# Token numbers from the chip, another order on SP's queue, fewer count reads, and one group's sums on VectorE, in a fused attention, expert and FFN kernel

## The reference

```python
def phi(x):                                  # x: batch 4, heads 8, seq 576, dim 64
    proj = einsum('bhsd,df->bhsf', x, w_phi)             # 128 features
    proj = proj - max(abs(proj), -1)
    return concatenate([exp(proj), exp(-proj)], -1)
kv = einsum('bhsf,bhsd->bhfd', phi(k), v); z = sum(phi(k), 2)
attn = phi(q) @ kv / (phi(q) . z + 1e-6)                 # -> x (2304, 512)

e_idx = argmax(x @ w_gate, 1)                            # one of 8 experts per token
out[e_idx == e] = softmax prob * sigmoid(x @ w_output_gate)[e] * (relu(x @ w1[e]) @ w2[e])   # 1024 wide

xn = x / sqrt(mean(x*x) + 1e-6) * rms_g                  # FFN, 1536 wide
y = (silu(xn @ w_gate) * (xn @ w_val)) @ w_out
```

## Time and profile before

| | |
|---|---|
| median of 3 runs | 870.38 us (868.96 to 873.25) |
| the profiled execution | 873.63 us, span of the trace 871.9 us |
| busy, share of the span | PE 96%, PEld 87%, DVE 62%, ACT 40%, POOL 19% |
| granted TensorE clock, mean | 0.998 |
| moved by DMA | 122.41 MB, 140 GB/s |

### The profile page before, as it was taken

The page is one execution under the profiler, slowest core; times in us unless marked ns, Lnnn a source line. Parts: engine busy times, 40 slices in busy tenths (PEclk is TensorE's granted clock), DMA queues, the critical chain, the costliest instruction groups (busy, mean ns, idle before and its releaser), DMA issues.

```text
span 871.9 us, 16594 instructions
## 1 busy us (share of the span) xinstructions
PE 840.2 (96%) x6216; PEld 757.3 (87%) x6217; DVE 538.9 (62%) x934; ACT 347.3 (40%) x547; POOL 161.4 (19%) x169
## 2 busy tenths in 40 slices
PE   8999999998988999999989999999999999999997
PEld 6685867767988999999989999999999998888885
DVE  5688786989766954445569777666765774212210
ACT  4544454573155533322354443333433443212211
POOL 1010302112350433203421031111110000101101
PEclk9999999999999999999999999999999999999999
DMA  8613713112349544554662852232421945343320
GB/s 285 209 57 138 275 54 108 55 38 75 127 175 267 227 114 97 141 148 150 184 230 77 280 180 79 79 80 79 142 71 54 357 150 184 123 139 125 125 101 36
DMA packets 65226, 122.41 MB, mean 140 GB/s; under 512 B 9200, under 2 KB 43120, under 8 KB 62480
## 3 DMA queue, kind: packets, MB, share of 16 engines
q1 hardware_dynamic: 57600, 91.98, 34.3%
q0 software_dynamic: 3488, 17.85, 5.3%
q10 hardware_dynamic: 4080, 11.80, 3.9%
HBM read 77.54 MB, written 44.09 MB: 139 GB/s over the span
## 4 chain that ended last, share of the span: by engine, by line
PE 78%; DVE 11%; issue 6%; DMA 2%; ACT 1%; DVEq 1%; SPq 0%; another core or an unknown queue 0%; POOLq 0%; POOL 0%; ACTq 0%
PE ps L1207 9%; PE ps L1209 9%; PE ps L1208 9%; PE ps L1259 5%; PE ps L1258 5%; PE ps L1260 5%; PE ps L956 3%; PE ps L1115 3%; PE ps L1116 3%; PE ps L1117 3%; PE ps L1128 3%; PE ps L1130 3%; PE ps L1129 3%; PE ps L1011 3%; PE ps L916 2%
## 5 line engine op out<-in xcount | busy, mean ns | idle before, releaser
L1207 PE MATMUL ps<-sH,tb 128*128 128x384 f32 x504 | 171.0, 339 | 5.9 <-DVE val L2018 2.9
L1208 PE MATMUL ps<-sL,tb 128*128 128x384 f32 x504 | 170.0, 337 | 0.0
L1209 PE MATMUL ps<-sH,tb 128*128 128x384 f32 x504 | 169.9, 337 | 0.0
L1207 PEld LDWEIGHTS ps<-sH,tb 128*128 128x128 f32 x504 | 95.0, 189 | 8.5 <-DVE val L2018 4.9
L1208 PEld LDWEIGHTS ps<-sL,tb 128*128 128x128 f32 x504 | 95.1, 189 | 0.1
L1209 PEld LDWEIGHTS ps<-sH,tb 128*128 128x128 f32 x504 | 95.2, 189 | 0.0
L2036 DVE TENSOR_TENSOR hTL<-h_st,hTH 128x768 fp32r<-128x768 f32 x36 | 33.0, 954 | 97.4 <-ACT hTH L1516 97.4
L1260 PE MATMUL ps<-woH,hTL 128*128 128x512 f32 x216 | 84.1, 389 | 0.0
L1259 PE MATMUL ps<-woL,hTH 128*128 128x512 f32 x216 | 84.1, 389 | 0.0
L1258 PE MATMUL ps<-woH,hTH 128*128 128x512 f32 x216 | 84.0, 389 | 0.0
L1115 PE MATMUL ps<-xmH,w1H 128*128 128x288 f32 x256 | 76.8, 300 | 5.9 <-issue 2.8
(11 more groups left out here) (246 smaller groups left out, 1784.8 us busy)
## 6 DMA issues: line engine op xcount, KB each, us to landing
h_dram<-hid SPq DMA_DIRECT2D x36, 384.0 KB, 2.8
h_st<-h_dram SPq DMA_DIRECT2D x18, 768.0 KB, 4.1
t_dram<-tb SPq DMA_DIRECT2D x6, 1792.0 KB, 5.7
t_raw<-in_ffn_up SPq DMA_DIRECT2D x13, 512.0 KB, 3.2
tb<-t_dram ACTq DMA_DIRECT2D x6, 1024.0 KB, 6.7
xin<-xs_dram SPq DMA_DIRECT2D x9, 578.2 KB, 9.3
xs_dram<-zrow SPq DMA_DIRECT2D x8, 578.2 KB, 7.9
qT<-in_q SPq DMA_DIRECT2D x4, 1152.0 KB, 5.8
```

What stands on the lines that cost most here:

```text
L1207: e.matmul(to, wh, xh, start=(fresh and c == 0), stop=False, skip_group_check=True)
L1208: e.matmul(to, wh, xl, start=False, stop=False, skip_group_check=True)
L1209: done = e.matmul(to, wl, xh, start=False, stop=(c == 1), skip_group_check=True)
```

## The change

1. Token numbers: `numbers_out` now takes the step's numbers from `xin` on the chip (96 partitions x 3 values of 4 bytes) instead of from `xs_dram`, as soon as the step's rows have been loaded. `rows_next` waits until the last numbers have been stored, since it overwrites `xin`. The two number transfers in the FFN's units 8 and 10 go.
2. SP's order in a step: rows in, FFN weights out, numbers out, normalised rows out, next FFN weights in.
3. Hand-over: group 0's rows are loaded ahead of the operands of visit 0; those of visit 1 wait for VectorE's first operand `s_hi0`. In unit 4 the last rows' store and group 2's load go ahead of the store of the unit's hidden rows.
4. Loop ends: counts of both turns are read at the head of a pair, and the first step (on VectorE also the next count) only inside a turn that has steps.
5. GpSimd loads the next raw `w1` ahead of `gate_rows`. Group 2's sums are VectorE's, in units 7 and 8.

```diff
+SUM_AT = {(1, "A"): ((1, 0), (1, 1)), (1, "B"): ((1, 2), (1, 3)), (7, "B"): ((2, 0), (2, 1)), (8, "A"): ((2, 2),),
+          (8, "B"): ((2, 3),)}
...
-        def turn_of(e, x):
-            tiles = e.value_load(tab[0:1, bass.ds(x + TILES, 1)], min_val=0, max_val=NTOK // G)
-            first = e.value_load(tab[0:1, bass.ds(x + FIRST, 1)], min_val=0, max_val=NTOK // G + E)
-            return tiles, first
+        def turns_of(e, pair):
+            return [e.value_load(tab[0:1, bass.ds(pair * 2 + (par + TILES), 1)], min_val=0, max_val=NTOK // G)
+                    for par in range(2)]
+        def first_of(e, x):
+            return e.value_load(tab[0:1, bass.ds(x + FIRST, 1)], min_val=0, max_val=NTOK // G + E)
...
             with e.Fori(0, pairs) as pair:
-                for par in range(2):
-                    tiles, first = turn_of(e, pair * 2 + par)
+                counts = turns_of(e, pair)
+                for par, tiles in enumerate(counts):
                     with e.If(tiles > 0):
+                        first = first_of(e, pair * 2 + par)
                         if once is not None:
                             once(pair, par)
...
+            def numbers_out(n, col):
+                e.wait_ge(s["ld"], n * 16 + 16)
+                settle(e, "carry_sp")
+                e.wait_ge(s["idst"], n * 16 + 16)
+                settle(e, "carry_sp")
+                with nc.allow_non_contiguous_dma(reason="token numbers"):
+                    e.dma_start(ids_dram[bass.ds(col, G), :].rearrange("(t p) a -> p t a", p=GR), xin[:, :, DM:DM + 1])\
+                        .then_inc(s["idst"], 16)
...
                 rows_in(x0 * REGION)
+                numbers_out(0, 0)
                 e.wait_ge(s["pe_XT"], KC)
+                e.wait_ge(s["idst"], 32)
                 rows_in(x0 * REGION + G)
...
                 row = row_of(n)
                 e.wait_ge(s["pe_XT"], n * KC)
                 settle(e, "carry_sp")
-                rows_in(row)
-            def numbers_out(n, col, row):
                 e.wait_ge(s["idst"], n * 16 + 16)
                 settle(e, "carry_sp")
-                with nc.allow_non_contiguous_dma(reason="token numbers"):
-                    e.dma_start(ids_dram[bass.ds(col, G), :], xs_dram[bass.ds(row, G), DM:DM + 1])\
-                        .then_inc(s["idst"], 16)
+                rows_in(row)
             def rows_out(n, col):
...
             with e.If(early < 1):
                 e.sem_inc(s["e_st"], 16)
                 rows_in(row_of(0))
+                numbers_out(0, column_of(0))
                 step_weights_in(0)
                 rows_next(1)
                 weights_out(0)
                 step_weights_in(1)
+            numbers_out(1, column_of(1))
             with e.Fori(0, total - 2) as n:
                 rows_next(n + 2)
                 weights_out(n + 1)
+                numbers_out(n + 2, column_of(n + 2))
+                rows_out(n, column_of(n))
                 step_weights_in(n + 2)
-                col, row = column_of(n), row_of(n)
-                rows_out(n, col)
-                numbers_out(n, col, row)
             rows_next(total)
...
             settle(e, "carry_sp")
-            e.wait_ge(s["e_st"], 16 * 8)
-            operands_in(0)
             e.wait_ge(s["xst"], total * 16)
             settle(e, "carry_sp")
             group_in(0)
-            prior_col, prior_row = column_of(prior), row_of(prior)
-            rows_out(prior, prior_col)
-            e.wait_ge(s["pe_s1"], total * FC)
-            settle(e, "carry_sp")
+            e.wait_ge(s["e_st"], 16 * 8)
+            operands_in(0)
+            rows_out(prior, column_of(prior))
+            e.wait_ge(s["s_hi0"], 1)
             operands_in(1)
             e.wait_ge(s["pe_s2"], total * FC + 2)
             settle(e, "carry_sp")
             group_in(1)
             e.wait_ge(s["s_lo"], 5)
             operands_in(2)
-            last_col, last_row = column_of(last), row_of(last)
+            last_col = column_of(last)
             for u in range(NU):
-                hidden_out(u)
                 if u == ROOT_AT + 1:
                     rows_out(last, last_col)
                     e.wait_ge(s["s_lo"], 7)
                     e.wait_ge(s["xst"], total * 16 + 32)
                     settle(e, "carry_sp")
                     group_in(2)
+                hidden_out(u)
                 for vis in MADE:
                     if last_of_visit(vis - 3) == u + 1:
                         weights_in(vis)
-                if u == 8:
-                    numbers_out(prior, prior_col, prior_row)
-                if u == 10:
-                    numbers_out(last, last_col, last_row)
                 if u == 15:
                     e.wait_ge(s["idst"], total * 16 + 16)
                     settle(e, "carry_sp")
...
             def split_step(pair, par, g):
                 add_squares(g - 1)
+                with e.If(has_turn(pair * 2 + (par + 2))):
+                    raw_in(1, pair * 2 + (par + 2), pair * (2 * PIECES) + ((par + 1) * PIECES + KC))
                 gate_rows(g + 1)
                 with e.If(has_turn(pair * 2 + (par + 2))):
-                    raw_in(1, pair * 2 + (par + 2), pair * (2 * PIECES) + ((par + 1) * PIECES + KC))
                     raw_in(2, pair * 2 + (par + 2), pair * (2 * PIECES) + (par + 2) * PIECES)
             e.wait_ge(s["tab_set"], 1)
...
-            e.wait_ge(s["s_lo"], 14)
-            row_sums(2, 0)
-            row_sums(2, 1)
...
                 with e.Fori(0, pairs) as pair:
-                    for par in range(2):
-                        tiles, first = turn_of(e, pair * 2 + par)
-                        nxt = e.value_load(tab[0:1, bass.ds(pair * 2 + (par + TILES + 1), 1)], min_val=0,
-                                           max_val=NTOK // G)
+                    counts = turns_of(e, pair)
+                    for par, tiles in enumerate(counts):
                         with e.If(tiles > 0):
+                            first = first_of(e, pair * 2 + par)
+                            nxt = e.value_load(tab[0:1, bass.ds(pair * 2 + (par + TILES + 1), 1)], min_val=0,
+                                               max_val=NTOK // G)
                             with e.Fori(0, tiles) as t:
                                 step(pair, par, first + t, nxt - t * (NTOK // G))
...
+                for sg, n in SUM_AT.get((u, pos), ()):
+                    row_sum(sg, n)
...
+            def row_sum(sg, n):
+                x, to, done = xst[sg], s_sum[sg], s[f"s_add{sg}"]
                 if n == 0:
+                    e.wait_ge(s[f"x_in{sg}"], 16)
+                    e.tensor_tensor(to[5][:, :, :], x[:, 0:2, GN:2 * GN], x[:, 2:4, GN:2 * GN], ALU.add).then_inc(done, 1)
                 if n == 1:
+                    e.wait_ge(done, 1)
+                    e.tensor_tensor(to[3][:, :, :], to[5][:, :, :], x[:, 0:2, 0:GN], ALU.subtract).then_inc(done, 1)
                 if n == 2:
+                    e.wait_ge(done, 2)
+                    e.tensor_tensor(to[2][:, :, :], x[:, 2:4, 0:GN], to[3][:, :, :], ALU.subtract).then_inc(done, 1)
+                if n == 3:
+                    e.tensor_tensor(to[4][:, :, :], x[:, 0:2, 0:GN], x[:, 0:2, GN:2 * GN], ALU.subtract).then_inc(done, 1)
...
                 beside(u, "A")
-                if u == 1:
-                    row_sums(0)
-                    row_sums(1)
                 if u == ROOT_AT:
                     mean(total - 1, BANKS[u % 2][3])
                 second_gate(u - 1)
-                if u == 1:
-                    row_sums(2)
-                    row_sums(3)
                 beside(u, "B")
```

More of the change, by code:

```diff
@@ L307, in build_program @@
             "FFN up weights of a step: loaded, sums, operands split, stored": "e_in e_add e_hi e_lo e_st",
-            "FFN rows loaded (one per group), their sums, operands split": "x_in0 x_in1 x_in2 s_add s_add1 s_hi0 s_hi s_lo",
+            "FFN rows loaded (one per group), their sums, operands split": "x_in0 x_in1 x_in2 s_add0 s_add1 s_add2 s_hi0 s_hi s_lo",
             "FFN up operands loaded (two parts per buffer)": "t_a0 t_a1 t_a2 t_b0 t_b1 t_b2",
@@ L460, in sums_done @@
         def sums_done(sg, n):
-            return (s["s_add1"], n) if sg == 1 else (s["s_add"], 4 * (sg // 2) + n)
+            return s[f"s_add{sg}"], n
         def nth_load(v):
@@ L692, in _ @@
                     e.wait_ge(s["s_lo"], 7 * NSG)
-                    e.wait_ge(s["s_add"], 8)
+                    e.wait_ge(s["s_add2"], 4)
                     e.dma_start(wo_st[0][:, :, :], ffn_out[:, 0:NF // 2, :]).then_inc(s["wo_in0"], 16)
```

35 lines of the change are left out of this document (11 added, 24 removed).

## The result

The changed kernel took 882.07 us (median, 878.53 to 883.84, 4 runs) against 869.74 us (868.96 to 873.25, 4 runs): ratio 1.0129, 95% interval 1.0086 to 1.0171. It is slower by 12.3 us, where 5.0 us less were forecast, and lies outside the range. The profiled execution took 882.51 us, with a span of 880.4.

What follows compares the result with a forecast made beforehand. TensorE, with work in 96% of the span, was taken to bound the kernel. Terms -1.5 + 0.7 - 0.6 - 2.7 - 0.9 = -5.0 us, from the median 870.38, gave 865.4 us, range 860.5 to 872.0.

Steps and rivals of the forecast that it cites:

- a: SP's order in a step: rows are stored earlier, TensorE's wait for `x2g` goes; -1.5 us (0 to -2.9).
- Rival 3: Numbers' transfer in front holds the next weights in each of six steps, `hmL` 1.6 us late; 876.5 us, chance 0.10.
- b: Loop ends: changed count reads alter TensorE's idle times in front of turns; +0.7 us (+0.3 to +0.8).
- d: Hand-over to the FFN: fewer reads, TensorE's 2.52 us idle falls to about 0.5, half clock goes; -2.7 us (-1.0 to -3.8).
- c: Group 0's rows loaded first: GpSimd's sums begin earlier, TensorE's 0.60 us idle at 441.26 goes; -0.6 us.
- e: Group 2's sums moved to VectorE, units 7 and 8: shortens TensorE's wait for `val`; -0.9 us (-1.5 to +1.5).
- rival 2: Group 2's rows land as late as before, VectorE stands 3.8 us in unit 7; 868.8 us, chance 0.08.

Runs made afterwards that it cites:

- the experiment that cures both: Changed kernel with unit 4's hidden rows stored first again and group 2's four sums all in unit 8 on VectorE; ratio 1.0079 to the kernel before.

## Why the prediction was wrong

**a (forecast -1.5 us; measured about +11.8).** This is the main step that failed, in the sentence "It starts when the weights' store ends (about 268.8), is through at 275, and the row store lands about 277.5, the next weights about 278.5, one us late for VectorE". I let the numbers' transfer follow a store that lands as before. In fact it is issued 1.4 us behind the store (257.51, 258.87) and runs beside it and beside the raw load, and the store itself lands after 19.6 us instead of 8.0. The next weights are issued at 277.33 and land about 287.1, 29.6 us behind the store's issue. I had them 17.6 behind it (278.5 and 260.87): 12.0 us too early. "GpSimd issues `w1raw` 2 us earlier [...]: nothing" failed with it: with the numbers in the middle this move costs 10.2 - 4.7 = 5.5 us of idle time. Worked out: 10.16 us of idle time against 1.83 + 1.06, so 7.3, and 4.5 for the half clock. The idea behind a may hold: with the numbers last and from DRAM, the rows' store ahead of the weights may be worth something. The medians' differences give 3.1 us in one comparison across series and 0.3 to 1.9 in another, the profiles next to nothing, so it stays open between 0 and 3.

Rival 3 named the mechanism, but I placed it in the wrong step. It had a late landing in each of six steps and six times 1.6 us. The landings are late in all of them (in the five later steps the next weights took 8.0 to 8.7 us, where they had taken 3.1 to 3.3), yet in this trace no step behind the first turn has an idle time of 0.35 us, but for the one of the reads. The whole loss is in the first turn, where the raw weights' loads are on the way as well. How thin the cover is shows in the run with the sums in unit 8, whose steps are those of the changed kernel. There one landing took 9.2 us, the sums met GpSimd's squares just as rival 3 says, and TensorE stood 1.26 us for `hmL` at 380.56:

```profile
375.35 0.69 DVE L1922 TENSOR_TENSOR t_raw<-t_raw 128x512 f32<-128x512 f32 x1
376.18 2.36 DVE L1926 TENSOR_TENSOR t_raw<-t_raw 128x256 f32<-128x256 f32 x1
```

The second of these takes 0.42 us in the changed kernel's trace. The rule that I cited there, from the Trainium skill's "DMA: Bandwidth & Descriptors" (Queues, rings and completion order), that a semaphore's increment lands only after every earlier write of that DMA engine, doesn't explain the store's 19.6 us by itself: the numbers were issued behind it. Where the raw load came late the trace agrees with it: what was issued behind the numbers landed after 12.8 and 13.0 us, the store in front of them after 6.8. The raw load's 16.6 us it leaves open, since that load went out ahead of the numbers. The page's other rule, read-modify-write below 512 B (Specifications), is tested by no run here: numbers from the chip and from DRAM held the store alike (19.6 and 18.5 us), but both are read and written in pieces of 4 bytes, so reading and writing are not told apart.

**b (forecast +0.7; measured +0.85 of idle time and 1.6 of clock).** The idle times are right: +0.80, +0.76 and -0.71 are +0.85, and the two longer ones are as before again when TensorE reads as before (1.58 and 0.47). But I put 0.7 us on top of an idle time of 1.57 and asked nothing about the clock, and the range stopped at +0.8. Behind the 2.37 us it fell to 1.2 GHz, so b is some +2.4 us. This term, mis-sized, is the second step that failed. "After idle times of 1.83 and 1.57 us the clock did not fall", which I used for d, is no rule either: in the run with the raw load late it fell behind 1.77 us (at 466.89; mean 0.58 in 468 to 470).

**c (-0.6).** Right. The idle time at the transposes is gone (with the reads alone, without the new order at the hand-over, 0.54 us stay). VectorE's normalisation took 3.30 us instead of 5.75 and not the 1.79 that I expected:

```profile
441.90 3.30 DVE L1809 SCALAR_TENSOR_TENSOR x2g<-x2g,gcol,rinv 128x288 f32<-128x288 f32 x4
```

**d (-2.7).** The mechanism is right and the size nearly. The 2.52 us fell to nothing, the half clock went (-1.6), and 0.84 us came at unit 1 (1.34 at 465.83, 0.50 in the trace of before). I had +0.9 there, for ScalarE's chain. What held it was the cover that I called thin, group 1's rows, for which ScalarE stood 2.47 us:

```profile
462.28 1.58 ACT L1480 ACTIVATE sH<-xst 128x768 fp32r<-128x768 f32 x2 [2.47 <-DMA xst<-xn_dram]
```

So d is -2.52 - 1.6 + 0.84 = -3.3 us. The reads alone bring the part at the hand-over, as argued.

**e (-0.9; measured about +5.4).** The third step that failed, with rival 2 as its likeness. Two sentences were wrong. "SP's new order (row store before the hidden rows of unit 4) moves the load some 2.8 us forward": the row store was issued 1.5 us behind ScalarE's weight loads (495.67), where it had been 4.2 behind them (492.65), and landed after 9.8 us instead of 6.5, so the load came at the same place in the unit or later (11.3 us behind those loads, 10.7 before). "The hidden store of unit 4, now behind that load, is wanted by ScalarE only two units later": it is, and it was 6.02 us late there. I had priced that wait at nothing without working out when the store would be issued. 5.29 - 1.54 = 3.75 us of idle time and 1.6 of clock make 5.4; the experiment that cures both gained 4.4 by the ratios and 6.1 in the units of its trace.

Together +11.8 + 2.4 - 0.6 - 3.3 + 5.4 = +15.7 us. Small idle times that no term names came out 1.0 us shorter. That makes 14.7, as by the list of idle times and clocks, beside 13.9 between the profiles from the first step on and 12.3 between the medians. Even with a at its forecast of -1.5 the sum would be +2.4.

## What to carry to other kernels

A transfer of many tiny writes is priced by what shares the engines with it, not by its own landing: before it is moved, list which big transfers will be on the way in its new place, in the first turns too, and put it last, where the queue next waits for something else anyway. When a store is put behind a waiting load on one queue, work out its new issue time and go to the engine that reuses its buffer; two late things behind one stall hide each other, so a cure of one shows nothing until the other is cured. An edit with a real gain (here the reads and the hand-over, c and d, some 4 us) can be found inside a slower kernel by putting its losing parts right one at a time. Whoever lengthens an idle time asks also whether the clock falls behind it. And where one stage varies by itself, as attention does here, compare the stages and not only the whole.

## What was unexpected of the hardware

- 288 writes of 4 bytes, 1.1 KB in all, issued 1.4 us behind a store of 1.8 MB, with a load of 2 MB issued 1.2 us ahead of it, made that store land in 19.6 us instead of 8.0. With the load alone it is 12.6 to 12.8 us. With the writes alone it is 6.8, and they hold what comes behind. Meanwhile the DMA engines showed as 95% busy at 73 GB/s. Where the bytes came from, the chip or DRAM, made no difference.
- Issued last of a step, the same writes are followed by a slow stretch, too (52 GB/s in the kernel before; without numbers in the steps the engines moved 393 and 360 GB/s in the two windows from 270 to 280), and it cost TensorE no more than the 1.83 us for `x2g` there.
- The granted clock of TensorE fell to 1.2 GHz in or behind every idle time of 2.83 us or more in steps and units. Below that either is seen. With 2.34 to 2.40 us in front of the first pair it fell in ten traces (the changed kernel's among them, 2.37) and not in two (2.36 and 2.38); it fell once each with 1.77 and 2.21 us, and did not with 1.83, 2.24 and 2.79.
- The time up to the steps differed by up to 9.9 us from one profiled execution to another (210.9 to 220.8), also between kernels that are alike up to there (210.9 in the changed kernel, 217.4 with group 2's sums in unit 8). That is more than most of the effects looked for.
